# Pooling in chunks of 500 points with a running maximum, and turned points kept in device memory

## The reference

```
h = mab(I, x)                    # I: 32 queries; softmax over 11456 points
x = mab(x, h)                    # softmax over 32 pooled rows, for every point
# mab(q, kv): s = q @ kv.T / sqrt(128); a = exp(s - max); a /= sum + 1e-9; a @ kv
# first layer: logits = normalized x @ normalized expert_emb / tau
# second layer: logits = x @ w_gate + modality_bias[modality_id]
# both: e = argmax(logits); out = softmax(logits)[e] * relu(x @ w1[e]) @ w2[e]
```

## Time and profile before

| what | value |
|---|---|
| median of 3 runs | 1140.99 us |
| span of the profiled execution (its first to its last instruction; no other time of it is given) | 1142.4 us |
| busy: PE, DVE, ACT, POOL | 94%, 69%, 63%, 14% |
| granted clock, mean | 0.973 |
| DMA, whole span | 52.89 MB, mean 46 GB/s |
| first pass of pooling, from the first turned group | 13.5 to 71.6 us |
| second pass | 75.4 to 125.0 us |
| products with pooled rows | 129.7 to 164.5 us |
| main loop | from 164.7 us |

### The profile page before, as it was taken

One profiled execution on the slowest core, in us unless ns is written; L12 is line 12 of the kernel. 1 busy time (PEld: TensorE's weight loads), 2 busy tenths in 40 slices (PEclk: granted clock), 3 DMA queues, 4 the chain that ended last, 5 costly groups with the idle time before them and its releaser, 6 DMA issues.

```text
span 1142.4 us, 29623 instructions
## 1 busy us (share of the span) xinstructions
PE 1074.0 (94%) x6715; PEld 610.7 (53%) x6715; DVE 789.5 (69%) x2342; ACT 724.2 (63%) x1761; POOL 160.9 (14%) x424
## 2 busy tenths in 40 slices
PE   6988876889999999999999999999999999999887
PEld 6987533445555555555555555555555555555443
DVE  4568884557776767777676777767677776767654
ACT  3458663456666666666666766666676666667553
POOL 3100001111111111111111111111111111111100
PEclk9989996889999999999999999999999999999999
DMA  8305650000000000000000000000000000000000
GB/s 332 120 22 163 212 174 21 12 21 27 27 27 27 27 26 20 26 27 27 27 27 27 19 27 27 27 27 27 27 20 26 27 27 27 27 27 18 12 22 20
DMA packets 38288, 52.89 MB, mean 46 GB/s; under 512 B 7504, under 2 KB 24056, under 8 KB 37604
## 3 DMA queue, kind: packets, MB, share of 16 engines
q1 hardware_dynamic: 38244, 52.35, 14.3%
HBM read 40.57 MB, written 11.78 MB: 46 GB/s over the span
## 4 chain that ended last, share of the span: by engine, by line
PE 91%; issue 3%; DVE 2%; ACT 1%; POOL 1%; DMA 1%; ACTq 0%; POOLq 0%; DVEq 0%
PE y L1196 41%; PE up L1219 22%; PE up L1209 7%; PE SM L1273 4%; PE TB L1116 3%; PE y L1092 2%; PE up L1084 2%; PE y L1288 2%; PE TB L1264 2%; PE up L1135 1%; PE TB L1243 1%; PE SM L1255 1%; PE up L1092 1%; PE TB L1231 1%; DMA stage<-in_moe_w 1%
## 5 line engine op out<-in xcount | busy, mean ns | idle before, releaser
L802 DVE SCALAR_TENSOR_TENSOR R<-up,R 128x500 f16<-128x500 f32 x736 | 491.0, 673 | 216.3 <-ACT R L552 216.2
L552 ACT ACTIVATE R<-up 128x500 f16<-128x500 f32 x736 | 416.1, 586 | 146.7 <-PE up L1209 79.1
L1219 PE MATMUL up<-R,W1B 128*128 (+1 forms) x1104 | 277.7, 382 | 21.1 <-issue 15.9
L1196 PE MATMUL y<-R 128*128 128x500 f16 x1104 | 292.1, 373 | 0.4 <-DVE R L802 0.4
L1196 PE MATMUL y<-R,W2A 128*128 128x500 f16 x1104 | 279.5, 375 | 1.3 <-DVE R L802 1.3
L1219 PEld LDWEIGHTS up<-R,W1B 128*128 x1104 | 108.8, 99 | 158.4 <-issue 49.5
L1196 PEld LDWEIGHTS y<-R,W2A 128*128 x1104 | 104.5, 101 | 101.1 <-issue 15.9
L1196 PEld LDWEIGHTS y<-R 128*128 x1104 | 100.3, 97 | 88.3 <-issue 3.1
L1209 PE MATMUL up<-R 128*128 (+1 forms) x368 | 138.3, 379 | 0.0
L485 POOL TENSOR_TENSOR st<-ss,root 125x4 f32<-125x4 f32 x46 | 46.8, 1018 | 386.0 <-ACT TB L584 386.0
L458 POOL CAST E<-ex 125x256 f16<-125x256 f32 x46 | 18.3, 397 | 403.7 <-ACT ex L603 403.7
(11 more groups left out here) (149 smaller groups left out, 1136.1 us busy)
## 6 DMA issues: line engine op xcount, KB each, us to landing
stage<-in_moe_w SPq DMA_DIRECT2D x24, 512.0 KB, 3.9
xin<-in_x SPq DMA_DIRECT2D x46, 250.0 KB
out<-SALL SPq DMA_DIRECT2D x46, 250.0 KB
R<-in_x SPq DMA_DIRECT2D x4, 2304.0 KB, 17.5
SALL<-in_moe_w SPq DMA_DIRECT2D x8, 512.0 KB, 4.3
R<-in_x SPq DMA_DIRECT2D x1, 2240.0 KB, 29.6
modi<-in_moe_modality_id SPq DMA_DIRECT2D x46, 3.9 KB
R<-in_x SPq DMA_DIRECT2D x1, 64.0 KB, 29.1
```

The source lines that it names most:

```text
L552: nc.scalar.activation(hhi[:, (u % UP) * CT:(u % UP + 1) * CT], ups[u % UP][:, 0:CT], ACT.Relu).then_inc(s["hi_done"], 1)
L802: nc.vector.scalar_tensor_tensor(hlo[:, o:o + CT], ups[u % UP][:, 0:CT], 0.0, hhi[:, o:o + CT], ALU.max, ALU.subtract).then_inc(s["lo_done ...
L1196: ins = mm(y[:, 0:CT], W[:, bass.ds(woff + (fb * 2 * C + o), C)], h[:, k * CT:(k + 1) * CT], start=opens and fb == 0 and n == 0, stop=fb = ...
L1219: ins = mm(ups[k][:, 0:CT], W1B[:, bass.ds(woff + (wl * F + fb * P), P)], ytb[:, bass.ds(yoff + yl * CW, CT)], start=n == 0, stop=n == 2)
```

## The change

The two passes become one. x is loaded in its 46 chunks, up to four of them (a round, `CHUNKS`) at a time, each in two DMAs of 120 and 5 partitions, into a ring of four rounds `xr`, with a column of ones behind each point. Each chunk is turned by TensorE (`turn_points`) and split into fp16 parts `xT`, the high one by ScalarE and the low one by VectorE; SP stores both to `x_turned` in device memory. `score_points` makes the scores of four chunks in fp16, three products each, with each chunk's 32 queries on 32 partitions of one bank of their own. VectorE takes the maximum with the one so far, which lies in the column behind the scores; ScalarE takes the exponential with this as bias, and the factor `alpha` for the older sum. TensorE turns the weights back (`turn_weights`), ScalarE copies them, `mix_points` multiplies them with the points and the ones in fp32, again each chunk on 32 partitions of its own, and VectorE adds that to `hacc` times `alpha`. At the end the four streams are weighed by their maxima and added by a product with `sel4`.

`W2A` is loaded whole and converted by GpSimd, in three steps for each expert. `W1B` is converted by ScalarE and VectorE behind pooling. The buffers that lay in `R` and `SALL` have tiles of their own. In the main loop the turning and its copy are gone: the load reads the two fp16 parts of a chunk from `x_turned` and waits for the scores of the chunk before; the scores are twelve fp16 products with the split `HT16`.

```diff
+    CHUNKS = [[b * NCB + g for g in range(q, min(q + STREAMS, NCB))] for b in range(NB) for q in range(0, NCB, STREAMS)]
+    NQ = len(CHUNKS)
 ...
+            def load_points(q):
+                for k, g in enumerate(CHUNKS[q]):
+                    r0 = row0(sp, g)
+                    slot = q % XR_N
+                    ready = s[f"x_loaded{slot * STREAMS + k}"]
+                    cutp = TQ // 8 * 8
+                    sp.dma_start(xr[0:cutp, slot, k, :, 0:C],
+                                 xf[r0:r0 + cutp * TJ, :].rearrange("(p j) c -> p j c", j=TJ)).then_inc(ready, 16)
+                    sp.dma_start(xr[cutp:TQ, slot, k, :, 0:C],
+                                 xf[r0 + cutp * TJ:r0 + CT, :].rearrange("(p j) c -> p j c", j=TJ)).then_inc(ready, 16)
+            sp.wait_ge(s["pads_cleared"], 1)
+            for q in range(XR_N):
+                load_points(q)
+            for e in range(NE):
+                sp.dma_start(as_w2(w2raw[:, e, :]), w2a[e, :, :].rearrange("(f p) c -> p f c", p=P)).then_inc(
+                    s[f"w2a_loaded{e // 2}"], 16)
+            for q in range(NQ):
+                for k, g in enumerate(CHUNKS[q]):
+                    slot = q % XT_N * STREAMS + k
+                    sp.wait_ge(s["lo_ready"], g + 1)
+                    sp.dma_start(XTD[g, :, :], xT[:, slot, :]).then_inc(s[f"x_stored{slot}"], 16)
+                if q >= 1 and q - 1 + XR_N < NQ:
+                    sp.wait_ge(s["mixed_in"], q)
+                    load_points(q - 1 + XR_N)
+            for e in range(NE):
+                if e >= 2:
+                    sp.wait_ge(s["w_lo_ready"], e - 1)
+                sp.dma_start(stage[:, e % 2, :], w1b[e, :, :]).then_inc(s[f"w_loaded{e % 2}"], 16)
 ...
+                sp.dma_start(xth[:, 0:2 * CT], XTD[bass.ds(q, 1), :, :].rearrange("a p n -> (a p) n")).then_inc(
                     s["chunk_loaded"], 16)
 ...
-                        sp.wait_ge(s["chunk_transposed"], c + 4)
+                        sp.wait_ge(s["chunk_scores"], c + 4)
 ...
+            for e in range(NE):
+                hi, lo, a = high_low(gp, "w2", W2A, e, w2raw[:, e, :])
+                gp.wait_ge(s[f"w2a_loaded{e // 2}"], 32)
+                nc.gpsimd.tensor_scalar(w2raw[:, e, :], w2raw[:, e, :], S_W, None, ALU.mult).then_inc(s["w2a_steps"], 1)
+                gp.wait_ge(s["w2a_steps"], 3 * e + 1)
+                nc.gpsimd.tensor_copy(hi, a).then_inc(s["w2a_steps"], 1)
+                gp.wait_ge(s["w2a_steps"], 3 * e + 2)
+                nc.gpsimd.tensor_tensor(lo, a, hi, ALU.subtract).then_inc(s["w2a_steps"], 1)
 ...
+            def high_points(g):
+                q, k = quad_of(g)
+                slot = q % XT_N * STREAMS + k
+                act.wait_ge(s["x_transposed"], g + 1)
+                if q >= XT_N:
+                    act.wait_ge(s[f"x_stored{slot}"], 16 * earlier(q, k, XT_N))
+                nc.scalar.activation(xT[:, slot, 0:CT], ups[g % 3][:, 0:CT], ACT.Copy, scale=S_X).then_inc(
+                    s["hi_ready"], 1)
+            def exp_points(q):
+                act.wait_ge(s["bias_made"], q + 1)
+                if q >= 2:
+                    act.wait_ge(s["p_transposed"], q - 1)
+                nc.scalar.activation(pex[:, q % 2, :], sbank(q)[:, 0:CT], ACT.Exp, bias=bias[:, q:q + 1],
+                                     scale=SCALE_I).then_inc(s["exp_ready"], 1)
+                nc.scalar.activation(alpha[:, q:q + 1], sbank(q)[:, CT:CT + 1], ACT.Exp, bias=bias[:, q:q + 1],
+                                     scale=SCALE_I).then_inc(s["alpha_ready"], 1)
+            def copy_points(q):
+                act.wait_ge(s["p_transposed"], q + 1)
+                if q >= 2:
+                    act.wait_ge(s["mixed_in"], q - 1)
+                nc.scalar.activation(pexT[:, q % 2, :], TB[0:TQ, :], ACT.Copy).then_inc(s["p_copied"], 1)
+            for g in CHUNKS[0]:
+                high_points(g)
+            for q in range(NQ):
+                nxt = CHUNKS[q + 1] if q + 1 < NQ else []
+                if q >= 1:
+                    copy_points(q - 1)
+                for g in nxt[0:2]:
+                    high_points(g)
+                exp_points(q)
+                for g in nxt[2:]:
+                    high_points(g)
+            copy_points(NQ - 1)
+            act.wait_ge(s["dve_setup_steps"], D_MNEG)
+            for b in range(NB):
+                nc.scalar.activation(mw[:, b:b + 1], mfin[:, b:b + 1], ACT.Exp, bias=mneg[:, b:b + 1],
+                                     scale=SCALE_I).then_inc(s["weights_ready"], 1)
+            act.wait_ge(s["w2a_steps"], 3 * NE)
+            for e in range(NE):
+                act.wait_ge(s[f"w_loaded{e % 2}"], 16 * (e // 2 + 1))
+                hi, _lo, a = high_low(act, "w1", W1B, e, stage[:, e % 2, :])
                 nc.scalar.activation(hi, a, ACT.Copy, scale=S_W).then_inc(s["w_hi_ready"], 1)
 ...
+            def low_points(g):
+                q, k = quad_of(g)
+                slot = q % XT_N * STREAMS + k
+                v.wait_ge(s["hi_ready"], g + 1)
+                nc.vector.scalar_tensor_tensor(xT[:, slot, CT:2 * CT], ups[g % 3][:, 0:CT], S_X, xT[:, slot, 0:CT],
+                                               ALU.mult, ALU.subtract).then_inc(s["lo_ready"], 1)
+            def maxima(q):
+                v.wait_ge(s["scores_done"], q + 1)
+                v.wait_ge(s["max_ready"], q + 1)
+                if q >= 1:
+                    v.wait_ge(s["alpha_ready"], q)
+                m = sbank(q + 1)[:, CT:CT + 1]
+                nc.vector.tensor_reduce(m, sbank(q)[:, 0:CT + 1], X, ALU.max).then_inc(s["final_steps"], 1)
+                v.wait_ge(s["final_steps"], q + 1)
+                nc.vector.tensor_scalar(bias[:, q:q + 1], m, -SCALE_I, None, ALU.mult).then_inc(s["bias_made"], 1)
+                if q % QB == QB - 1:
+                    v.wait_ge(s["bias_made"], q + 1)
+                    nc.vector.tensor_copy(mfin[:, q // QB:q // QB + 1], m).then_inc(s["final_ready"], 1)
+                    if q + 1 < NQ:
+                        v.wait_ge(s["final_ready"], q // QB + 1)
+                        nc.vector.memset(m, -3.0e38).then_inc(s["max_ready"], 1)
+                else:
+                    v.sem_inc(s["max_ready"], 1)
+            def accumulate(q):
+                b, rows = q // QB, M * len(CHUNKS[q])
+                v.wait_ge(s["mixed_in"], q + 1)
+                v.wait_ge(s["alpha_ready"], q + 1)
+                if q >= 1:
+                    v.wait_ge(s["acc_ready"], q)
+                nc.vector.scalar_tensor_tensor(hacc[0:rows, b, :], hacc[0:rows, b, :], alpha[0:rows, q:q + 1],
+                                               y2[0:rows, 0:C + 1], ALU.mult, ALU.add).then_inc(s["acc_ready"], 1)
 ...
+            def turn_points(g):
+                q, k = quad_of(g)
+                pe.wait_ge(s[f"x_loaded{q % XR_N * STREAMS + k}"], 32 * (earlier(q, k, XR_N) + 1))
+                if g >= 3:
+                    pe.wait_ge(s["lo_ready"], g - 2)
+                for j in range(TJ):
+                    ins = nc.tensor.transpose(ups[g % 3][:, j * TQ:(j + 1) * TQ], xr[0:TQ, q % XR_N, k, j, 0:C],
+                                              ident[0:TQ, 0:TQ])
                 ins.then_inc(s["x_transposed"], 1)
+            def score_points(q):
+                pe.wait_ge(s["lo_ready"], CHUNKS[q][-1] + 1)
+                pe.wait_ge(s["max_ready"], q + 1)
+                if q >= 1:
+                    pe.wait_ge(s["bias_made"], q)
+                if q >= 2:
+                    pe.wait_ge(s["alpha_ready"], q - 1)
+                for n, (il, xl) in enumerate(((0, 0), (1, 0), (0, 1))):
+                    for k in range(len(CHUNKS[q])):
+                        ins = mm(sbank(q)[k * M:(k + 1) * M, 0:CT], ind16[:, il, :],
+                                 xT[:, q % XT_N * STREAMS + k, xl * CT:(xl + 1) * CT], start=n == 0, stop=n == 2)
                 ins.then_inc(s["scores_done"], 1)
+            def turn_weights(q):
+                pe.wait_ge(s["exp_ready"], q + 1)
+                if q >= 1:
+                    pe.wait_ge(s["p_copied"], q)
+                for j in range(TJ):
+                    ins = nc.tensor.transpose(TB[0:TQ, j * P:(j + 1) * P], pex[:, q % 2, j * TQ:(j + 1) * TQ],
+                                              ident[:, :])
+                ins.then_inc(s["p_transposed"], 1)
+            def mix_points(q):
+                pe.wait_ge(s["p_copied"], q + 1)
+                if q >= 1:
+                    pe.wait_ge(s["acc_ready"], q)
+                for j in range(TJ):
+                    for k, g in enumerate(CHUNKS[q]):
+                        rows = TQ if j < CT - STEP or g % NCB == NCB - 1 else TQ - 1
+                        ins = mm(y2[k * M:(k + 1) * M, 0:C + 1], pexT[0:rows, q % 2, j * P + k * M:j * P + (k + 1) * M],
+                                 xr[0:rows, q % XR_N, k, j, :], start=j == 0, stop=j == TJ - 1)
```

(38 more changed lines are left out.)

402 lines of the change are left out of this document (137 added, 265 removed).

## The result

The changed kernel takes 1133.01 us (median of 8 runs, 1130.38 to 1135.10) against 1141.01 us (median of 8, 1136.51 to 1146.67). The ratio is 0.9926, with a 95% interval of 0.9901 to 0.9951. It is faster, by 8 us or 0.7%, where 47.5 us were forecast; the forecast's range of 1074 to 1128 doesn't hold it. The profiled execution took 1135.07 us, its span 1133.3 us at a mean clock of 0.95.

The account below looks back on a forecast made before the run. The prediction took TensorE to bound the kernel, at 91% of the chain of waits. Gains of 11.5 (up to the main loop), 4.5 (filling steps) and 31.5 (steady steps) made 47.5 us, from 1140.99 to 1093.5; range 1074 to 1128.

Parts of the forecast that it names:

- Part 3: Pooling in one pass: the DMAs set rounds of 5.7 us, and pooling ends at 86.7 instead of 125.
- The forecast's own sign of being wrong: Pooling ending after 105 us, or a steady main-loop step staying above 19.6 us.
- Rivals B: Pooling: DMAs run at 430 GB/s, the chain of 4.5 us sets the round; 1080 us; chance 0.12.
- C: Pooling: 512-byte pieces and unspread part loads starve it; decides from rounds of about 9.8 us; 1171 us; chance 0.09.
- The drain at a change of tiling mode: Pooling's rounds on TensorE: each mode change drains the engine, several times a round; added to 4.0 us without a size.
- Rival A: Pooling: four products don't share the array, or the clock stays low; rounds 8.5 or about 8 us; 1125; chance 0.18.
- Part 4: Weight conversion once hidden by pooling: first weight product 29.6 us behind pooling, main-loop scores at 153.2 against 164.7.
- rival D: Under pooling: GpSimd's conversion of W2A takes twice as long, ending at 115 instead of 75; 1120 us; chance 0.07.
- 12 us of cover: Under pooling: the time left between W2A's conversion on GpSimd, done by 75, and pooling's end at 86.7.
- Part 1: Steady main-loop step: gains 0.75 us, VectorE's low halves setting 5.43 us before layer 1; 42 steps give 31.5 us.
- Rival E: Main loop: no speedup, narrow products cost as the fp32 ones did; 1107 us; chance inside the forecast's 0.50.
- Part 2: Steps that fill the main loop's pipeline: transposes, copy and cheaper scores gain 4.5 us (ends 1 and 6).

Follow-up runs that it names:

- Experiments 2: Plain rows: changed kernel with point rows lacking the column of ones, sums from 16 more one-column products a round; 1100.34 us, ratio 0.9622 to the kernel before.
- experiment 6: Changed kernel with the source read so a partition's four rows lie 120 (or 5) apart, both sides cut; 1116.46 us, ratio 0.977.
- 5: Changed kernel with point rows of 160 floats instead of 129, each beginning at a multiple of 128 bytes; 1131.72 us, ratio 0.9905.
- Experiment 1: Changed kernel with W2A's loads issued two at a time behind the point loads of rounds 1 to 4; 1132.06 us, ratio 0.988.
- Experiment 10: Changed kernel without the column of ones, W1B converted inside rounds 4 to 11, one W2A load in each of rounds 0 to 7; 1093.34 us, ratio 0.9572.
- experiment 8: Changed kernel with one expert of W1B loaded, split and kept in each of pooling's rounds 4 to 11; 1120.1 us, ratio 0.9795.
- experiment 11: Changed kernel with four fp32 transposes put back on TensorE in each main-loop step, result unused; 1140.33 us, ratio 0.9992.
- 12: Changed kernel with the four transposes and also ScalarE's copy of 500 columns, with TensorE's wait for it, put back; 1140.96 us, ratio 0.9994.

## Why the forecast was wrong, by its own steps

**Part 3, the step that failed: "SP has 12 issues in a round at 0.33 each, 4.0 us. So the DMAs set the round".** The 0.33 was read from a load that is whole on both sides. The new load writes four rows of 512 bytes with a gap of four bytes between them from a whole 2048-byte piece, and its issue took 0.85 us, that of the five last partitions 0.76. With eight of these and four stores a round costs SyncE 8.9 to 10.3 us, and the rounds were 9.07 us in the mean instead of 5.7. Experiments 2 and 6 show it (the issue is short when both sides are whole, and when both are cut), and 5 excludes the rows' alignment to 128 bytes. The forecast's own sign of being wrong, pooling ending after 105, came.

The last scores stood at 123.92 instead of 80.2, 44 us late. Of this the six rounds from 64.23 to 118.64 make 20 us, and the one long round from 29.51 to 56.77 makes 22; the four others make 2.

A short issue would not have given 5.7 us either. The 290 to 430 GB/s at full share were read from rows of before, and experiment 6 showed 276 with pieces of 512 bytes and rounds of 7.13 us. So of the 3.1 us by which a round of the changed kernel exceeds that of plain rows, the issue makes 1.9 (9.07 to 7.13), and the length of the pieces 1.2 (7.13 to 5.95), as far as experiment 6 parts them.

Rivals B and C spoke of the DMAs, which stood at 0.69. C's point of decision, a round of about 9.8 us, was not reached in the mean, nor its price of 1171. Its mechanism, starving by short pieces, is real but worth 1.2 us a round, not 4.

**Part 3, the round that I forecast exists, in another layout.** With plain rows it is 5.95 us in the mean, where 5.7 were forecast, at full share, 338 GB/s, inside the 290 to 430 assumed; without stores it is 4.93, the chain forecast at 4.5. The array is shared: twelve score products of 500 columns held TensorE from 17.72 to 18.47, 0.75 us, and in the next round 0.65 (22.99 to 23.64), where one after the other they would take 2.5. The Trainium skill (TensorEngine Tiling (Array Packing), Theoretical Speedup) gives up to four times for 32 columns; the trace agrees, with 3.3 to 3.8 times. The drain at a change of tiling mode, which the prediction took from the same page (Tiling Modes), can't be told apart in these times. The clock didn't stay low through pooling either: 0.87 from 60 to 120 us, though 0.62 from 30 to 60. Rival A falls. The first scores came at 17.72 (forecast 17.5).

**A second miss: W2A's eight loads stood in no sum.** I gave them neither issue time nor bytes; SyncE was held 12.1 us by them in the changed kernel and 18.9 with plain rows, and the first stores wait behind. Experiment 1 shows that in the changed kernel moving them was worth only 3 us. With plain rows pooling's last products ended at 99.4, not 86.7, and this is again one long round:

```profile
27.86 0.82 PE L1099 MATMUL up<-GW,ind 128*32 128x500 f16 x12
...
47.85 1.44 PE L1099 MATMUL y<-GW,ind 128*32 128x500 f16 x12
```

It takes 19.99 us, 14 more than forecast. W2A's 4.2 MB at the 329 GB/s of that kernel from 30 to 60 us are 13 us, an estimate. Experiment 10 fits it, since spreading the loads over the rounds moved the mark by only 2.3 us; no experiment took these bytes away.

**Part 4 held.** From the end of the last products (128.9) to the first weight product it is 26.8 us (forecast 29.6), and to the main loop's scores 35.9 more (forecast 36.9). GpSimd took 48.4 us for W2A, as forecast (40 to 50), so rival D falls. But it began at 37.3, since SyncE issued the loads only from 30.3 on, and ended at 85.7, not before 80. It lay under pooling because pooling ended at 128.9; of the 12 us of cover that I counted, a pooling that ended at 86.7 would have left 1. That this exposed stretch was worth taking away shows in experiment 8: 13 us. The cost that I put there so was real, and a design that hides it beats the change.

**Part 1 held in size and in mechanism.** 0.71 us a step against 0.75. VectorE's floor between router and layer 1 is 5.52 instead of 5.43, which from 6.18 gives 0.66 of it (experiment 11); ScalarE's copy was free (12). What was removed is so: scores 0.81 to 0.30 when TensorE doesn't wait (269.75 to 270.05), 0.51 us; the transposes 0.14; 0.06 is not accounted for. Rival E falls.

**Part 2 and the tail.** The steps that fill the pipeline gained 15.1 us instead of 4.5, and the end lost 6.7. Part of both is time in which TensorE waited for nothing that the profile shows. In the filling steps before, these waits took 3.50 us at 217.15 and 4.71 at 243.38; after, 3.01 at 237.40 and none in the next step. In the tail they went from 7.6 to 11.8 us in all. In each of these waits of over 2 us the queue that the profile names "instruction" moved a packet, and from 300 to 1000 us it moved none, in both kernels. That fits waits for the program's own instructions; no experiment tried it, and the rest of both differences stays open.
